# Four diagonal tiles for the first four head pairs, and two averages of v earlier in VectorE's order

## The chip, the cores and the metric

The kernel runs on one core of a Trainium2 chip. The metric is the device time of one execution in microseconds (us). TensorE (PE) multiplies matrices and loads its weights (PEld); VectorE (DVE), ScalarE (ACT) and GpSimd (POOL) do the elementwise work; SyncE (SP) issues every transfer. Each engine works through its own list of instructions in order, and the engines wait for each other by semaphores.

## The reference

Attention for 4 batches, 8 heads, 576 positions and a head size of 64, followed by two layers over the 2304 tokens:

```python
# down-sampled attention: means of 4 positions, softmax, each output repeated 4 times
q_d, k_d, v_d = (t.reshape(B, H, Sd, 4, D).mean(axis=3) for t in (q, k, v))
out_up = np.repeat(sm_attn(q_d, k_d, v_d), 4, axis=2)
# local attention: only keys with |i - j| < 4
scores = np.where(mask, scale * q @ k.T, -1e9)
out_local = softmax(scores) @ v
x = (out_up + out_local) as (2304, 512)
# first layer, 512 -> 1536 -> 512
x = (silu(x @ w_gate) * (x @ w_val)) @ w_out
# second layer, 512 -> 2048 -> 512, negative hidden values scaled by alpha
return g(x @ w_in) @ w_out2
```

## The kernel before, in words

The tokens go in 8 blocks of 288 through the attention and the first layer, then in 6 blocks of 384 through the second layer. Matrix products take each operand as a high part (rounded) and a low part (the rest), and add three products (`products`, L1005, and `outputs`, L1025). In the first layer, the attention of block j+1 is woven between the products of block j. The attention of block 0 has nothing to hide behind: it is the head of the kernel, written out by hand for each engine ("mode 0"). It takes four pairs of heads, k = 0 to 3. The change lies in this head alone.

For pair k, the head does the following:

- PE multiplies the local scores (L904) and the scores of the averaged q and k (L912, after VectorE's `average_qk`, L673).
- VectorE finds maxima and subtracts them (`local_maxima`, L697 and L701; `down_maxima`, L710 and L712). ScalarE takes the exponentials (L509, L516).
- VectorE forms the sums and their reciprocals (`reciprocals`: L718, L721, L725, the last counts `inv_ready`). GpSimd then multiplies both kinds of weights by them (`normalise`, L456 and L459; it waits for `inv_ready`).
- VectorE turns the local weights in 32 x 32 blocks into a tile `turned` that has four key groups on its diagonal and zeros elsewhere (`turn_local`, L739, four instructions). The zeros come from a memset (L659) at the start. PE transposes the averaged weights (L942), and ScalarE copies them (`copy_down_t`, L525).
- PE forms the outputs: 12 matmuls of `turned` with v's windows (L956), then 8 of the copied weights with the averaged v (L967, which counts `att_ready`). The averages of v are VectorE's for pairs 0 and 1 (`average_v`, L684) and GpSimd's for pairs 2 and 3 (L468, L470).
- VectorE adds both outputs into x (`add_up`, L748 and L750), ScalarE rounds x to its high part (L529), and the low part is GpSimd's for pairs 0 to 2 (`split_x_lo`, L474) and VectorE's for pair 3 (L755). The products of block 0 (L1005) begin when all four high and low parts are there: PE waits for GpSimd's three (`x_lo_early`, L997) and then for VectorE's (`x_lo_ready`).

Before, `turned` has two buffers for the four pairs, `turned_one` and `turned_alone`, used in turn. So VectorE's `turn_local` of pair 2 waits until PE has finished pair 0 (`att_ready` 1), and that of pair 3 until PE has finished pair 1.

What sets the order in the head is each engine's written list. VectorE's is printed in the diff below. GpSimd's is: the two weight pieces 0 and 1; `normalise(0)`; `normalise(1)`; `average_v(2)`; `normalise(2)`; `normalise(3)`; `average_v(3)`; low part of piece 2 (L437); then `split_x_lo(0)`, low part of piece 3, `split_x_lo(1)`, low part of piece 4, `split_x_lo(2)`, low part of piece 5. PE's is: scores of the four pairs; transposes 0 and 1; outputs 0; transposes 2; outputs 1; transposes 3; outputs 2; outputs 3. ScalarE's is: exponentials of the four pairs; `copy_down_t(0)`; piece 2; `copy_down_t(1)`; x high 0; `copy_down_t(2)`; piece 3; x high 1; `copy_down_t(3)`; piece 4; x high 2 and 3; piece 5.

SP issues, in this order: q and k of four pairs (`load_qk`, L293); weight pieces 0 to 2 (L304); v of four pairs, for each first the source of the averages (`load_vsrc`, L299) and then the windows (`load_vwin`, L296); pieces 3 and 4; alpha; then the refills for block 1. The source of v for block 1 goes into pair 0's buffer and waits for the first `v_averaged`; the windows wait for `att_ready`; each further weight piece j waits until piece j-3 has been split (`w_ready`).

The head's own buffers lie over the later part of the split weights `w_hi`. `EARLY_HI` pieces of `w_hi` are kept clear ahead of them; ScalarE fills the pieces behind during block 0.

Of the kernel before, what the change touches and what calls it, by code (L numbers as in the profile page):

```python
# [23 lines left out]
PAIRS = HEADS // 2  # L24
TILES = 3
TQ = TB // TILES
GROUPS = 4
GQ = TQ // GROUPS
SCORED = GQ
GK = 32  # L30
# [26 lines left out]

POOL_PIECES = 2
EARLY_PIECES = 6
EARLY_HI = 14  # L60
POOL_AVERAGES = 2
BANK = 512
STEPS1 = NB * C1
# [16 lines left out]
def build(nc, qk, vwin, vsrc, w1, w2, alpha, out, y_t):  # L80
    with ExitStack() as ctx:
        def sem(name):
            return ctx.enter_context(nc.semaphore(name))

        def sb(name, shape, dt=F32, where=ctx):
            return where.enter_context(nc.sbuf_tensor(name, shape, dt))
# [21 lines left out]
        def local_both(mode, k):  # L108
            n = scores_ps[mode][k][0]
            return ps[:, n * BANK:(n + 2) * BANK].rearrange("p (e b) -> p e b", e=2)[:, :, 0:DOWN].rearrange("p e (t c) -> p e t c", c=GK)  # L110
# [14 lines left out]
        with ExitStack() as early:  # L125
            sb("first_pieces", [128, EARLY_HI, PIECE], where=early)
            qk_early = [sb(f"qk_early{k}", [128, QK_W], where=early) for k in range(2, PAIRS)]
            vwin_early = [sb(f"vwin_early{k}", [128, TILES, 2 * HEAD], where=early) for k in range(2, PAIRS)]
            vsrc_early = [sb(f"vsrc_early{k}", [HQ, 2, 2 * HEAD, FACTOR], where=early) for k in range(1, PAIRS)]
            qk_d_early = [sb(f"qk_d_early{k}", [128, AVERAGED], where=early) for k in range(1, PAIRS)]  # L130
            v_d_early = [sb(f"v_d_early{k}", [HQ, 2, 2 * HEAD], where=early) for k in range(1, PAIRS)]
            local_early = [sb(f"local_early{k}", [128, 2 * TILES, GK], where=early) for k in range(1, PAIRS)]
            down_early = [sb(f"down_early{k}", [HQ, 2, SEQ_D], where=early) for k in range(1, PAIRS)]
            x_f32_early = [sb(f"x_f32_early{k}", [128, TB], where=early) for k in range(1, PAIRS)]
            band_tmp = sb("band_tmp", [128, GROUPS, GK], BF16, where=early)
            ident_bf = sb("ident_bf", [128, 128], BF16, where=early)
            first_max = sb("first_max", [128, PAIRS, STATS], where=early)
            first_neg = sb("first_neg", [HQ, PAIRS, 2], where=early)
            first_sum = sb("first_sum", [128, PAIRS, STATS], where=early)
            first_padded = sb("first_padded", [128, PAIRS, STATS], where=early)  # L140
            first_inv = sb("first_inv", [128, PAIRS, STATS], where=early)
# [15 lines left out]
        with ExitStack() as alone:  # L157
            turned_alone = sb("turned_alone", [128, 2 * TILES, GROUPS, GK], where=alone)
# [8 lines left out]
        with ExitStack() as att:  # L167
# [9 lines left out]
            turned_one = sb("turned_one", [128, 2 * TILES, GROUPS, GK], where=att)  # L177
# [14 lines left out]
        v_d = ([v_d_one] + v_d_early, [v_d_one] * PAIRS)  # L192
        local = ([local_one] + local_early, [local_one] * PAIRS)
        down = ([down_one] + down_early, [down_one] * PAIRS)
        turned = ([turned_one, turned_alone] * 2, [turned_one] * PAIRS)
        down_t = ([down_t_one, down_t_alone] * 2, [down_t_one] * PAIRS)
        x_f32 = ([x_f32_one] + x_f32_early, [x_f32_one] * PAIRS)

        def slot_of(k, mode):

            return k % 2 if mode else k
# [28 lines left out]
        turned_zeroed = sem("turned_zeroed")  # L230
# [16 lines left out]
        att_ready = sem("att_ready")  # L247
# [407 lines left out]

        @block.vector
        def _(dve):
            for n, buffer in enumerate((turned_one, turned_alone)):
                nc.vector.memset(buffer[:, :, :, :], 0.0).then_inc(turned_zeroed, 1)  # L659
            for mode in range(2):  # L660
                nc.vector.memset(row_sum[mode][:, :, :], 0.0).then_inc(scalars_ready, 1)
# [14 lines left out]
            def average_v(a, k):  # L676
                q = PAIRS * a + k
                mode = 0 if isinstance(a, int) and a == 0 else 1
                if mode:
                    dve.wait_ge(vsrc_in[0], 16 * (q - PAIRS) + 32)  # L680
                    dve.wait_ge(att_ready, q)
                else:
                    dve.wait_ge(vsrc_in[k], 16)
                nc.vector.tensor_reduce(v_d[mode][k][:, :, :], vsrc_sb[mode][k][:, :, :, :],  # L684
                                        AX_X, ALU.add).then_inc(v_averaged, 1)

            def local_maxima(a, k, half, mode):

                q, slot = PAIRS * a + k, slot_of(k, mode)
                dve.wait_ge(scores_ready, q + 1)  # L690
                s = local_both(mode, k)
                found = row_max[mode][:, slot, 0:2 * TILES].rearrange("p (e t) -> p e t", e=2)
                if mode:
                    b = band[:, half:half + 1, :, :].to_broadcast([128, 2, TILES, GK])
                    nc.vector.tensor_tensor(s, s, b, ALU.add).then_inc(masked, 1)
                    dve.wait_ge(masked, q - PAIRS + 1)
                nc.vector.tensor_reduce(found, s, AX_X, ALU.max).then_inc(local_max_found, 1)  # L697
                dve.wait_ge(local_max_found, q + 1)
                if mode:
                    dve.wait_ge(local_turned, GROUPS * q)  # L700
                nc.vector.tensor_tensor(local[mode][k][:, :, :].rearrange("p (e t) c -> p e t c", e=2), s,  # L701
                                        found.unsqueeze(3).to_broadcast([128, 2, TILES, GK]), ALU.subtract).then_inc(shifted, 1)

            def down_maxima(a, k, mode):

                q, slot = PAIRS * a + k, slot_of(k, mode)
                if mode:
                    dve.wait_ge(down_ready, q)
                found = row_max[mode][0:HQ, slot, 2 * TILES:STATS]
                nc.vector.tensor_reduce(found, down_both(mode, k), AX_X, ALU.max).then_inc(down_max_found, 1)  # L710
                dve.wait_ge(down_max_found, q + 1)
                nc.vector.tensor_scalar(neg_max[mode][:, slot, :], found, -SCALE / FACTOR ** 2, None, ALU.mult).then_inc(neg_max_ready, 1)  # L712

            def reciprocals(a, k, mode):

                q, slot = PAIRS * a + k, slot_of(k, mode)
                dve.wait_ge(local_ready, q + 1)
                nc.vector.tensor_reduce(row_sum[mode][:, slot, 0:2 * TILES], local[mode][k][:, :, :], AX_X, ALU.add).then_inc(summed, 1)  # L718
                dve.wait_ge(summed, q + 1)
                dve.wait_ge(down_ready, q + 1)  # L720
                nc.vector.tensor_scalar(row_padded[mode][:, slot, :], row_sum[mode][:, slot, :], 1e-9, None, ALU.add).then_inc(sum_padded, 1)  # L721
                dve.wait_ge(sum_padded, q + 1)
                if mode:
                    dve.wait_ge(down_normed, q)
                nc.vector.reciprocal(row_inv[mode][:, slot, :], row_padded[mode][:, slot, :]).then_inc(inv_ready, 1)  # L725

            def turn_local(a, k, mode):

                q = PAIRS * a + k
                dve.wait_ge(local_normed, q + 1)  # L730
                if mode:
                    dve.wait_ge(att_ready, q)
                elif k >= 2:
                    dve.wait_ge(att_ready, q - 1)
                else:
                    dve.wait_ge(turned_zeroed, 2)
                for i in range(GROUPS):
                    rows = slice(GK * i, GK * i + GK)
                    nc.vector.transpose(turned[mode][k][rows, :, i, :], local[mode][k][rows, :, :]).then_inc(local_turned, 1)  # L739
# [42 lines left out]
            down_maxima(0, 2, 0)  # L782
            reciprocals(0, 1, 0)
            turn_local(0, 0, 0)
            local_maxima(0, 3, 0, 0)
            down_maxima(0, 3, 0)
            reciprocals(0, 2, 0)
            turn_local(0, 1, 0)
            reciprocals(0, 3, 0)
            average_v(0, 0)  # L790
            turn_local(0, 2, 0)
            average_v(0, 1)
            add_up(0, 0, 0)
            turn_local(0, 3, 0)
            add_up(0, 1, 0)
# [344 lines left out]
```

## Time and profile before

| | |
|---|---|
| median of 3 runs | 978.19 us (976.51 to 978.28) |
| the profiled execution's own time | 977.23 us |
| its span in the profile | 975.2 us |
| PE busy | 948.9 us, 97% |
| PE weight loads busy | 886.3 us, 91% |
| VectorE busy | 547.8 us, 56% |
| ScalarE busy | 247.7 us, 25% |
| GpSimd busy | 138.7 us, 14% |
| largest entry in the chain of waits | PE, products at L1005, 50% |

The profile is that of one execution. Times in its rows are us from the span's start, and the second number of a timeline row is how long the row was busy. The difference of 2.0 us between its time and its span lies outside the recorded instructions.

### The profile page before, as it was taken

Reading aid. Unit: us, or ns where it says so; the run is one execution under the profiler, and the core shown is the slowest. Engines: PE = TensorE matmul, PEld = TensorE weight load, DVE = VectorE, ACT = ScalarE, POOL = GpSimd, SP = SyncE. Lnnn points to the kernel's source line nnn. Section 1 sums busy time; section 2 is a strip of 40 time slices with the busy share of each in tenths; the row PEclk is TensorE's granted clock in tenths of the full one; section 3 lists DMA queues with packets and bytes.
Section 4 is the critical chain, followed back from the end, with each engine's and each line's share of the span. In section 5 each row is a group of like instructions: output and inputs, shape, how many; then the busy total and the mean of one; then the engine's idle time right before and its main releaser. Section 6 shows DMA issues by size and latency. Waiting matters only on the chain.

```text
span 975.2 us, 20383 instructions
## 1 busy us (share of the span) xinstructions
PE 948.9 (97%) x7912; PEld 886.3 (91%) x7912; DVE 547.8 (56%) x1166; ACT 247.7 (25%) x631; POOL 138.7 (14%) x158
## 2 busy tenths in 40 slices
PE   4799999999999999999999999999999999999998
PEld 3789999899998999999999999999999999999997
DVE  7677666665765767666663544445445444444433
ACT  2455222222222222222224531111111111111111
POOL 6677010010000000010104840000000000000000
PEclk9999999999999999999999999999999999999999
DMA  8465212211211322222106530010010100100000
GB/s 257 130 193 167 85 58 60 83 53 48 94 48 41 94 66 70 59 66 72 43 10 198 163 101 1 1 66 1 0 65 0 64 1 0 65 0 0 32 0 32
DMA packets 31735, 63.06 MB, mean 65 GB/s; under 512 B 2993, under 2 KB 14257, under 8 KB 31665
## 3 DMA queue, kind: packets, MB, share of 16 engines
q1 hardware_dynamic: 31664, 62.02, 20.7%
q8 instruction: 57, 0.93, 0.4%
q14 instruction: 14, 0.11, 0.0%
HBM read 52.57 MB, written 9.44 MB: 64 GB/s over the span
## 4 chain that ended last, share of the span: by engine, by line
PE 90%; DVE 3%; POOL 2%; DMA 2%; issue 1%; ACT 1%; SPq 0%; DVEq 0%; ACTq 0%; POOLq 0%
PE ps L1005 50%; PE ps L1042 20%; PE ps L1025 14%; PE ps L956 2%; PE ps L904 1%; POOL w_lo L437 1%; DMA w_raw<-w 1%; PE ps L912 1%; PE ps L967 1%; PE ps L942 1%; DMA qk<-qk 0%; DVE x_lo L755 0%; DVE qk_d_early L673 0%; DVE turned_one L739 0%; DVE turned_alone L739 0%
## 5 line engine op out<-in xcount | busy, mean ns | idle before, releaser
L1005 PE MATMUL ps<-x_hi,w_hi 128*128 128x288 f32 x768 | 232.9, 303 | 5.8 <-issue 3.2
L1005 PE MATMUL ps<-x_lo,w_hi 128*128 128x288 f32 x768 | 227.1, 296 | 0.0
L1005 PE MATMUL ps<-x_hi,w_lo 128*128 128x288 f32 x768 | 226.4, 295 | 0.0
L579 ACT CAST h_hi<-hidden 128x288 fp32r<-128x288 f32 (+1 forms) x192 | 90.8, 473 | 404.4 <-DVE hidden L869 331.9
L832 DVE TENSOR_TENSOR h_lo<-hidden,h_hi 128x288 fp32r<-128x288 f32 (+1 forms) x192 | 112.5, 586 | 75.8 <-ACT h_hi L579 72.5
L1005 PEld LDWEIGHTS ps<-x_hi,w_hi 128*128 128x128 f32 x768 | 144.4, 188 | 10.2 <-issue 3.6
L867 DVE TENSOR_SCALAR gated<-ps,alpha_sb 128x384 f32<-128x384 f32 x96 | 59.3, 618 | 159.4 <-PE ps L1005 159.4
L1005 PEld LDWEIGHTS ps<-x_hi,w_lo 128*128 128x128 f32 x768 | 144.9, 189 | 0.0
L1005 PEld LDWEIGHTS ps<-x_lo,w_hi 128*128 128x128 f32 x768 | 144.8, 189 | 0.0
L1025 PE MATMUL ps<-h_hi,w_hi 128*128 128x288 f32 x384 | 115.5, 301 | 0.1
L1042 PE MATMUL ps<-w_lo,h_hi 128*128 128x512 f32 x288 | 113.2, 393 | 0.0
L1042 PE MATMUL ps<-w_hi,h_lo 128*128 128x512 f32 x288 | 113.2, 393 | 0.0
L1025 PE MATMUL ps<-h_hi,w_lo 128*128 128x288 f32 x384 | 112.8, 294 | 0.0
L1025 PE MATMUL ps<-h_lo,w_hi 128*128 128x288 f32 x384 | 112.7, 294 | 0.0
L1042 PE MATMUL ps<-w_hi,h_hi 128*128 128x512 f32 x288 | 112.2, 389 | 0.4 <-DVE h_lo L832 0.4
L437 POOL TENSOR_TENSOR w_lo<-w_raw,w_hi 128x512 fp32r<-128x512 f32 x68 | 90.2, 1338 | 43.7 <-ACT w_hi L574 27.4
L842 DVE SCALAR_TENSOR_TENSOR gated<-gated,ps 128x288 f32<-128x288 f32 x96 | 43.4, 452 | 90.9 <-ACT gated L604 90.9
L604 ACT ACTIVATE gated<-ps 128x288 f32<-128x288 f32 x96 | 39.4, 410 | 175.5 <-PE ps L1005 175.4
L847 DVE SCALAR_TENSOR_TENSOR hidden<-gated,ps 128x288 f32<-128x288 f32 x96 | 43.6, 454 | 52.0 <-PE ps L1005 50.7
L1025 PEld LDWEIGHTS ps<-h_hi,w_hi 128*128 128x128 f32 x384 | 72.1, 188 | 0.6 <-issue 0.6
L1025 PEld LDWEIGHTS ps<-h_lo,w_hi 128*128 128x128 f32 x384 | 72.2, 188 | 0.0
L1025 PEld LDWEIGHTS ps<-h_hi,w_lo 128*128 128x128 f32 x384 | 72.1, 188 | 0.0
(127 smaller groups left out, 1424.4 us busy)
## 6 DMA issues: line engine op xcount, KB each, us to landing
w_raw<-w SPq DMA_DIRECT2D x68, 256.0 KB, 2.7
qk<-qk SPq DMA_DIRECT2D x30, 436.0 KB, 3.4
vsrc_one<-vsrc SPq DMA_DIRECT2D x29, 288.0 KB
vwin<-vwin SPq DMA_DIRECT2D x30, 192.0 KB, 2.3
y_t<-y_sb SPq DMA_DIRECT2D x8, 576.0 KB, 3.4
x_raw<-y_t SPq DMA_DIRECT2D x6, 768.0 KB, 5.6
out<-y_sb SPq DMA_DIRECT2D x5, 768.0 KB, 4.0
qk_early<-qk SPq DMA_DIRECT2D x2, 436.0 KB, 6.4
```

Of the source, the lines that this page charges most:

```text
L437: nc.gpsimd.tensor_tensor(w_lo[:, at, :], raw, w_hi[:, at, :].bitcast(F32), ALU.subtract).then_inc(w_ready, 1)
L579: nc.scalar.copy(h_hi[r][:, 0:width], hidden[r][:, 0:width]).then_inc(h_hi_ready, 1)
L604: nc.scalar.activation(gated[:, 0:TB], gate_ps, ACT.Tanh, scale=0.5).then_inc(tanh_ready, 1)
L832: nc.vector.tensor_tensor(h_lo[r][:, 0:width], hidden[r][:, 0:width], h_hi[r][:, 0:width].bitcast(F32), ALU.subtract).then_inc(h_lo_ready, 1)
L842: nc.vector.scalar_tensor_tensor(out=gated[:, 0:TB], in0=gated[:, 0:TB], scalar=1.0, in1=gate_ps, op0=ALU.add, op1=ALU.mult).then_inc(gate ...
L847: nc.vector.scalar_tensor_tensor(out=hidden[r][:, 0:TB], in0=gated[:, 0:TB], scalar=0.5, in1=val_ps, op0=ALU.mult, op1=ALU.mult).then_inc( ...
L867: nc.vector.tensor_scalar(gated[:, :], pre_ps[r], 0.0, alpha_sb[:, c:c + 1], ALU.min, ALU.mult).then_inc(gated_ready, 1)
L904: last = nc.tensor.matmul(local_ps(mode, k, e)[GK * i:GK * i + SCORED, t * GK:(t + 1) * GK], qk_sb[mode][k][rows, first:first + SCORED], q ...
L956: nc.tensor.matmul(o[rows, t * TQ:(t + 1) * TQ].rearrange("p (i q) -> p i q", q=GQ), vwin_sb[mode][k][:, t, rows], turned[mode][k][:, e * ...
L1005: mm = nc.tensor.matmul(out_ps, w[:, piece, 128 * k:128 * k + 128], x_parts[low][:, k, :], start=(k == 0 and n == 0), stop=(k == KC - 1 an ...
L1025: mm = nc.tensor.matmul(y_ps[m], w[:, piece, 128 * m:128 * m + 128], (h_lo if low else h_hi)[c % 2][:, 0:TB], start=(c == 0 and n == 0), s ...
L1042: mm = nc.tensor.matmul(banks[m], (h_lo if low else h_hi)[c % 2][:, 128 * m:128 * m + 128], w[:, piece, :], start=(c == 0 and n == 0), sto ...
```

## The change

Pairs 2 and 3 get diagonal tiles of their own (`turned_early`), so `turn_local` no longer waits for `att_ready` in the head; VectorE zeroes four tiles instead of two. The two tiles of 128 x 768 f32 lie in the head's region, which now begins at piece 12 of `w_hi` instead of 14. VectorE's `average_v(0, 0)` moves from behind `reciprocals(0, 3, 0)` to right behind `turn_local(0, 0, 0)`, and `average_v(0, 1)` from behind `turn_local(0, 2, 0)` to right behind `turn_local(0, 1, 0)`. The lists of the other engines are as before.

```diff
-EARLY_HI = 14
+EARLY_HI = 12
...
+            turned_early = [sb(f"turned_early{k}", [128, 2 * TILES, GROUPS, GK], where=early) for k in range(2, PAIRS)]
...
-        turned = ([turned_one, turned_alone] * 2, [turned_one] * PAIRS)
+        turned = ([turned_one, turned_alone] + turned_early, [turned_one] * PAIRS)
...
-            for n, buffer in enumerate((turned_one, turned_alone)):
+            for buffer in turned[0]:
                 nc.vector.memset(buffer[:, :, :, :], 0.0).then_inc(turned_zeroed, 1)
...
                 if mode:
                     dve.wait_ge(att_ready, q)
-                elif k >= 2:
-                    dve.wait_ge(att_ready, q - 1)
                 else:
-                    dve.wait_ge(turned_zeroed, 2)
+                    dve.wait_ge(turned_zeroed, PAIRS)
...
             turn_local(0, 0, 0)
+            average_v(0, 0)
             local_maxima(0, 3, 0, 0)
             down_maxima(0, 3, 0)
             reciprocals(0, 2, 0)
             turn_local(0, 1, 0)
+            average_v(0, 1)
             reciprocals(0, 3, 0)
-            average_v(0, 0)
             turn_local(0, 2, 0)
-            average_v(0, 1)
             add_up(0, 0, 0)
             turn_local(0, 3, 0)
             add_up(0, 1, 0)
```

## Rows read from the trace of the kernel before

**Rows 1.** The page's head: span of the profiled execution.
```profile
span 975.2 us, 20383 instructions
```
**Rows 2.** Windows of PE: stretch, length, busy (instructions), clock, DMA share, GB/s.
```profile
40.00:330.00 290.00, 284.29 (x3099) 1.00 0.29 88
```
**Rows 3.** Timeline of PE, products of block 0: first, twelfth, and two later ones.
```profile
33.53 0.58 PE L1005 MATMUL ps<-x_hi,w_hi 128*128 128x288 f32 x1 [2.48 <-DVE x_lo L755]
...
36.30 0.44 PE L1005 MATMUL ps<-x_hi,w_lo 128*128 128x288 f32 x1
...
42.12 0.29 PE L1005 MATMUL ps<-x_hi,w_hi 128*128 128x288 f32 x1
42.26 0.29 PE L1005 MATMUL ps<-x_lo,w_hi 128*128 128x288 f32 x1
```
**Rows 4.** Timeline of VectorE, 0 to 6 us; in brackets idle time and its releaser.
```profile
1.79 0.70 DVE L659 MEMSET turned_alone<- 128x768 f32 x1
...
4.04 1.06 DVE L673 TENSOR_REDUCE qk_d_one<-qk 128x217 f32<-128x868 f32 x1 [1.48 <-DMA qk<-qk]
...
5.73 1.06 DVE L673 TENSOR_REDUCE qk_d_early<-qk 128x217 f32<-128x868 f32 x1 [0.63 <-DMA qk<-qk]
```
**Rows 5.** Timeline of VectorE, 16.5 to 25 us.
```profile
16.56 0.36 DVE L697 TENSOR_REDUCE first_max<-ps 128x6 f32<-128x192 f32 x1
...
17.70 0.17 DVE L712 TENSOR_SCALAR first_neg<-first_max 72x2 f32<-72x2 f32 x1
...
18.16 0.17 DVE L721 TENSOR_SCALAR first_padded<-first_sum 128x8 f32<-128x8 f32 x1
...
20.64 0.20 DVE L725 RECIPROCAL first_inv<-first_padded 128x8 f32<-128x8 f32 x1
20.76 1.16 DVE L684 TENSOR_REDUCE v_d_one<-vsrc_one 72x256 f32<-72x1024 f32 x1
22.92 1.57 DVE L739 STREAM_TRANSPOSE turned_one<-local_early 32x192 f32<-32x192 f32 x4 [1.00 <-PE ps L967]
24.52 1.22 DVE L684 TENSOR_REDUCE v_d_early<-vsrc_early 72x256 f32<-72x1024 f32 x1
```
**Rows 6.** Timeline of VectorE, 25 to 33.7 us.
```profile
27.16 1.57 DVE L739 STREAM_TRANSPOSE turned_alone<-local_early 32x192 f32<-32x192 f32 x4 [0.79 <-PE ps L967]
...
32.32 0.85 DVE L755 TENSOR_TENSOR x_lo<-x_f_early,x_hi 128x288 fp32r<-128x288 f32 x1 [0.50 <-ACT x_hi L529]
```
**Rows 7.** Timeline of GpSimd, 18 to 34 us.
```profile
18.76 1.04 POOL L468 TENSOR_TENSOR vsrc_early<-vsrc_early 72x512 f32<-72x512 f32 x1 [2.47 <-DMA vsrc_early<-vsrc]
19.88 0.63 POOL L470 TENSOR_TENSOR v_d_early<-vsrc_early 72x256 f32<-72x256 f32 x1
...
21.56 0.51 POOL L456 TENSOR_TENSOR local_early<-local_early,first_inv 128x192 f32<-128x192 f32 x1
...
26.91 0.79 POOL L474 TENSOR_TENSOR x_lo<-x_f,x_hi 128x288 fp32r<-128x288 f32 x1 [1.27 <-ACT x_hi L529]
...
30.04 0.80 POOL L474 TENSOR_TENSOR x_lo<-x_f_early,x_hi 128x288 fp32r<-128x288 f32 x1 [1.04 <-ACT x_hi L529]
...
32.07 0.79 POOL L474 TENSOR_TENSOR x_lo<-x_f_early,x_hi 128x288 fp32r<-128x288 f32 x1
32.89 1.42 POOL L437 TENSOR_TENSOR w_lo<-w_raw,w_hi 128x512 fp32r<-128x512 f32 x1
```
**Rows 8.** Timeline of all engines at 10.5 us: GpSimd and VectorE side by side.
```profile
10.53 1.26 POOL L437 TENSOR_TENSOR w_lo<-w_raw,w_hi 128x512 fp32r<-128x512 f32 x1
10.75 1.07 DVE L721 TENSOR_SCALAR first_padded<-first_sum 128x8 f32<-128x8 f32 x1
```
**Rows 9.** Transfers issued in 5.8 to 6.3 and 6.8 to 7.2 us: KB, us to landing.
```profile
vwin<-vwin SPq DMA_DIRECT2D x1, 192.0 KB, 9.0
...
vwin<-vwin SPq DMA_DIRECT2D x1, 192.0 KB, 10.2
```
**Rows 10.** Timeline of all engines: the weight pieces 5 and 6 being issued.
```profile
25.67 3.68 SPq L304 DMA_DIRECT2D w_raw<-w x2
```

## The prediction, made before the changed kernel ran

> **What bounds the kernel now.** I read the page first. The span is 975.2 us [rows 1]. The windows of PE come next: between 40 and 330 us PE is busy for 284.29 of 290 us [rows 2], so behind the head PE sets the time, and a head that ends earlier or later moves all that follows. What the change can be worth is therefore when the products of block 0 start. That is the first row of PE's timeline: 33.53 us, after 2.48 us idle, released by VectorE's low part of pair 3 [rows 3]. That part ended at 32.32 + 0.85 = 33.17 [rows 6], 0.36 us ahead of the matmul. GpSimd's third low part ended at 32.07 + 0.79 = 32.86 [rows 7]. So two engines end the head, and the second is only 0.31 us ahead of the first. That margin matters more here than VectorE's idle time.
>
> VectorE's timeline shows what the change aims at: 1.00 us idle before the turn of pair 2 and 0.79 us before that of pair 3, both released by PE's outputs [rows 5, 6]. From the turn of pair 3 on the head is one chain: the turn ends at 28.73 (27.16 + 1.57) and, with the 0.03 us that separate 22.92 + 1.57 from 24.52 [rows 5], at 28.76 VectorE adds up pair 1, ScalarE rounds it and then copies the weights of pair 3, PE forms the outputs of pair 3, VectorE adds them up, and the low part follows. From 28.76 to 33.17 that is 4.41 us, which moves as a whole.
>
> **The change, part by part.**
>
> Two more memsets: 2 x 0.70 = 1.40 us and two short gaps on VectorE [rows 4]. What hides them is the wait of 1.48 us for q and k at 4.04. At most some 0.15 us sticks out, and the next wait of 0.63 us for a transfer swallows that [rows 4]. Cost: nothing. Moving the region by two pieces costs nothing either: those pieces are written by ScalarE inside block 0, well behind 33.53.
>
> The two waits for a free tile go: up to 1.00 + 0.79 = 1.79 us of VectorE's time. The averages are only moved, so VectorE's work until pair 1 is added up is the same. Without other waits that step would begin at 28.76 - 1.79 = 26.97, and VectorE's last low part would end at 33.17 - 1.79 = 31.4.
>
> The first moved average starts at 16.56, where pair 3's maxima began [rows 5]. Its data are there: the windows of pair 0, issued behind its source on the same queue, landed 9.0 us after an issue before 6.3, so by 15.3; those of pair 1 by 7.2 + 10.2 = 17.4, ahead of the second average [rows 9]. It takes 1.16 us, and everything behind it on VectorE is that much later: pair 3's maxima, the exponentials that ScalarE does before any copy, and the reciprocals of pair 2. The second average (1.16 to 1.22 us [rows 5]) delays the reciprocals of pair 3 further. These were ready at 20.64 + 0.20 = 20.84; now 20.84 + 1.16 + 1.22 = 23.22 at the earliest.
>
> **Who waits for that** is GpSimd's normalise of pair 3, which began at 21.56 [rows 7]. With less than 0.1 us for the signal (an estimate, from the gaps of that size between instructions) it can begin at 23.3, 1.74 us later. Behind it in GpSimd's list stand the average of pair 3, piece 2 and the three low parts that PE needs. On the way GpSimd has two idle stretches, 1.27 and 1.04 us, both for ScalarE's rounding [rows 7], which itself comes earlier or no later. They absorb 2.31 us. So GpSimd's third low part would end at 32.86 + 1.74 - 2.31 = 32.29, and it, not VectorE, would be last.
>
> **The port between VectorE and GpSimd** decides the rest. VectorE's scalar step L721, 0.17 us elsewhere [rows 5], took 1.07 us at 10.75 and ended at 11.82, just behind GpSimd's subtraction that ran from 10.53 to 11.79 [rows 8]. After the move, the same kind of step for pair 3 (L712) comes at 17.70 + 1.16 = 18.86 [rows 5]. GpSimd's first step of the average of pair 2 starts at 18.76, released by a transfer, and runs until 19.80 [rows 7]. The transfer does not move, so L712 runs into it and ends at about 19.82 instead of 19.03: 0.80 us. L721 then comes at about 20.1, beside GpSimd's second step, which ends at 19.88 + 0.63 = 20.51 [rows 7]: another 0 to 0.35, I take 0.3. That is the likeliest course: VectorE's chain moves by 1.79 - 1.1 = 0.7 us to the front, the last low part of VectorE ends near 32.5, and the reciprocals of pair 3 come at 23.22 + 1.1 = 24.3. Normalise starts at 24.4, 2.8 us late, 0.5 more than the 2.31 us absorb. GpSimd's third low part then ends at 32.86 + 0.5 = 33.4. VectorE's low part (two SBUF inputs) falls beside these steps; where they met before, GpSimd's next subtraction took 1.42 us against 1.26 [rows 7, 8], so 0 to 0.2 more. With 0.36 us until the matmul the products start at 33.7 to 33.9, 0.2 to 0.4 us later than before; with the lower bound of every term (0.6 of port waits) they start at 33.2. I take +0.3 us.
>
> The Trainium skill (SBUF — State Buffer, Who interferes with whom) says that issue order, not the op's shape, decides who blocks. L712 is only 0.10 us behind GpSimd's step by the sum above. If the transfer lands 0.1 us later, L712 goes first, and by that rule GpSimd loses only the short step; that is rival B.
>
> **Transfers.** The source of v for block 1 waits for the first average to read its buffer, and is now issued about 4.2 us earlier (20.76 to 16.56 [rows 5]). It lies behind the early transfers on one queue, so it delays no load of the head. Piece 5 was issued at 25.67 [rows 10], when piece 2 had been split; GpSimd splits that up to 2.8 us later, so it is issued at 28.5. It still lands ahead of its use, which is ScalarE's last copy of the head, behind the high part of pair 3 (before 32.32). With the 3.68 us of that row for both pieces, 32.2 for the second is the worst. Cost: nothing, and up to 0.3 if the cover fails.
>
> **The clock at the start.** The first products are slow: 33.53 to 36.30 for eleven steps is 0.25 us each, the lower level (1.2 GHz), against 0.14 at 42.12, the upper (2.4 GHz) [rows 3]; PE had mostly idled before. If the rise comes at the same moment, whatever the start, a shift of the start counts only 0.14 / 0.25 = 0.56.
>
> **The sum.** 977.23 for the profiled execution + 0.3 = 977.5. The median of the runs is 0.96 above that execution, the lowest run 0.72 below it; I put the forecast at 977.8, between the sum and the same sum made on the median. A measurement of this kernel can tell some 0.2%, 1.96 us, from no change; nothing above comes near it.
>
> **The rivals.**
> A, the forecast (0.52): GpSimd ends the head, start between 33.2 and 33.9, no change that can be told; 977.8.
> B (0.25): L712 gets the port first. GpSimd loses 0.17 us, and only L721 stands, for about 0.4. Normalise of pair 3 starts at 23.7, 2.1 us late, inside the 2.31 that are absorbed; GpSimd ends at 32.7 to 32.9, VectorE at 31.8, products at 33.05 to 33.3. That is 0.2 to 0.5 us gained against before, 0.65 less than A: 977.15. For it speaks the margin of 0.10 us, against it that L712 is behind in the sum.
> C (0.12): the idle time of VectorE is all gained, because GpSimd takes its waits elsewhere or meets no port wait. Bounds: 31.4 + 0.36 gives 31.76, a gain of 1.77 us; with GpSimd last at 32.29 it is 0.9 us. Against the 977.5 that stands for no change in the forecast that is 975.7 to 976.6, and with a low run under it faster by more than 1.96 us. Against it speaks GpSimd's order, where `normalise(3)` stands ahead of all three low parts.
> D, slower (0.11): the late normalise costs nearly its full amount and the clock rises late. Place: GpSimd's row at 21.56 [rows 7]. If only its idle 1.27 absorbs and not the 1.04, its third low part ends at 32.86 + 2.8 - 1.27 = 34.4, and the products start at 34.8, 1.2 us slower; with 1 us more at the lower level of the clock, which costs 1 - 0.56 = 0.44, that is 1.7 us: 979.2. It decides from the point where ScalarE's rounding of pair 1 moves back together with GpSimd. To pass 1.96 the clock would have to stay low for 1.8 us more. Against it: VectorE adds up pair 1 earlier, not later.
>
> **How the numbers follow.** The range holds A and B with the spread of the runs (976.51 to 978.28, so 0.9 to either side of their middle), the nearer part of C, and D to its price: 976.0 to 979.3. Faster by over 0.2% takes C and a low run, or part of B with one: 0.08. Slower by over 0.2% takes D and more: 0.05. Within: 0.87.
>
> **What would show it.** Right: no idle before the turns of pairs 2 and 3; L712 of pair 3 at 18.8 to 18.9 with about 0.9 us; reciprocals of pair 3 at about 24; GpSimd idle before `normalise(3)` and next to none before its low parts; PE's first product released by GpSimd's L474, at 33.2 to 33.9; from there on the trace as before. Wrong: the first product still released by VectorE, or before 32.8; L712 at 0.17 us (then B or C); an idle stretch of PE behind 40 us that was not there.

## The result, and the profile after

The changed kernel takes 980.08 us (median of 13 runs, 979.24 to 982.92), the kernel before 978.33 us (median of 13, 976.51 to 979.97). The ratio is 1.0019, with a 95% interval of 1.0011 to 1.0028: it is slower, by some 1.9 us (by the ratio; the medians differ by 1.75). The forecast was no change, with a range that ended at 979.3.

The page's head and parts of its costliest groups; [rows 1] answers to the first line.

```profile
span 979.6 us, 20385 instructions
PE 951.7 (97%) x7912; PEld 888.0 (91%) x7912; DVE 552.9 (56%) x1168; ACT 247.9 (25%) x631; POOL 138.7 (14%) x158
...
L1004 PE MATMUL ps<-x_hi,w_hi 128*128 128x288 f32 x768 | 233.7, 304 | 10.2 <-DVE x_lo L754 6.0
```

The last line shows where to look: PE's products waited 6.0 us for VectorE's low part of x, where before that wait was 2.48 us [rows 3]. The lines of the changed kernel are numbered otherwise: L754 is before's L755, L1004 is L1005, L738 is L739, and on GpSimd L469, L475 and L438 are L468, L474 and L437.

VectorE's timeline in the head, to be set beside [rows 5, 6]:

```profile
15.14 1.53 DVE L738 STREAM_TRANSPOSE turned_one<-local_one 32x192 f32<-32x192 f32 x4
16.70 1.22 DVE L685 TENSOR_REDUCE v_d_one<-vsrc_one 72x256 f32<-72x1024 f32 x1
...
18.97 0.21 DVE L713 TENSOR_SCALAR first_neg<-first_max 72x2 f32<-72x2 f32 x1
...
19.47 0.43 DVE L722 TENSOR_SCALAR first_padded<-first_sum 128x8 f32<-128x8 f32 x1
...
23.33 0.20 DVE L726 RECIPROCAL first_inv<-first_padded 128x8 f32<-128x8 f32 x1
23.45 1.53 DVE L738 STREAM_TRANSPOSE turned_early<-local_early 32x192 f32<-32x192 f32 x4
25.01 0.23 DVE L747 TENSOR_SCALAR up<-ps 128x72 f32<-128x72 f32 x1
25.28 0.46 DVE L749 TENSOR_TENSOR x_f<-ps,up 128x288 f32<-128x288 f32 x1
25.66 1.56 DVE L738 STREAM_TRANSPOSE turned_early<-local_early 32x192 f32<-32x192 f32 x4
27.25 0.23 DVE L747 TENSOR_SCALAR up<-ps 128x72 f32<-128x72 f32 x1
...
29.85 0.46 DVE L749 TENSOR_TENSOR x_f_early<-ps,up 128x288 f32<-128x288 f32 x1
30.81 4.36 DVE L754 TENSOR_TENSOR x_lo<-x_f_early,x_hi 128x288 fp32r<-128x288 f32 x1 [0.50 <-ACT x_hi L530]
```

Both idle stretches ahead of the turns are gone. Pair 1 is added up at 27.25 instead of 28.77, and the low part of pair 3 is ready to go at 30.81 instead of 32.32. So far the change does what it says: it brings the last step 1.5 us forward. That step then takes 4.36 us instead of 0.85. The instruction ahead of it (29.85), of the same size but with only one of its two inputs in SBUF, took its usual 0.46 us beside GpSimd's work.

GpSimd's timeline, to be set beside [rows 7], shows what stood beside it:

```profile
18.12 1.03 POOL L469 TENSOR_TENSOR vsrc_early<-vsrc_early 72x512 f32<-72x512 f32 x1 [1.69 <-DMA vsrc_early<-vsrc]
...
23.61 0.51 POOL L457 TENSOR_TENSOR local_early<-local_early,first_inv 128x192 f32<-128x192 f32 x1 [2.27 <-DVE first_inv L726]
...
29.64 0.79 POOL L475 TENSOR_TENSOR x_lo<-x_f_early,x_hi 128x288 fp32r<-128x288 f32 x1
30.39 1.27 POOL L438 TENSOR_TENSOR w_lo<-w_raw,w_hi 128x512 fp32r<-128x512 f32 x1
31.62 0.79 POOL L475 TENSOR_TENSOR x_lo<-x_f_early,x_hi 128x288 fp32r<-128x288 f32 x1
32.37 2.48 POOL L438 TENSOR_TENSOR w_lo<-w_raw,w_hi 128x512 fp32r<-128x512 f32 x2
```

The normalise of pair 3 starts at 23.61, 2.05 us later than before, and after it GpSimd has no idle stretch left until 32.37 + 2.48 = 34.85. VectorE's low part ends at 30.81 + 4.36 = 35.17, 0.32 us behind that. Before, GpSimd's third low part ended at 32.86, and VectorE's ended at 33.17, 0.31 us behind it [rows 6, 7].

PE's timeline, to be set beside [rows 3]:

```profile
35.52 0.58 PE L1004 MATMUL ps<-x_hi,w_hi 128*128 128x288 f32 x1 [5.98 <-DVE x_lo L754]
...
40.66 0.34 PE L1004 MATMUL ps<-x_hi,w_lo 128*128 128x288 f32 x1
40.84 0.29 PE L1004 MATMUL ps<-x_hi,w_hi 128*128 128x288 f32 x1
```

The first product comes 1.99 us later, which is about the measured difference. This one profiled execution took longer than the median (981.4 us), its span is 4.4 us over that of before, and the clock explains part of the rest. The products of 0.44 us, the lower level, went on until 40.8, 5.3 us from the first one, against less than 4.4 us before (they took 0.29 us, the upper level, from 37.87). At the start of a later block the changed kernel was 3.1 us behind (313.62 against 310.51), after PE had idled there for 2.23 us against 1.43. Then this execution had one more stretch at the lower level, here beside the same stretch of before:

```profile
313.70:317.00 3.30, 3.30 (x16) 0.52 0.02 5
```
```profile
313.70:317.00 3.30, 3.30 (x27) 1.00 0.03 5
```

These are windows of PE (length, busy time, instructions, granted clock, DMA share, GB/s). At 0.52 of full speed PE did 16 products in 3.3 us where it did 27 before, so the stretch costs some 1.3 us (an estimate from these two rows), which completes the 4.4. Nothing makes it a cost of the change: 5 of the 13 runs of the changed kernel report a mean clock below 1, and so do 24 of the 74 runs of the kernel before that were taken beside the experiments (an outlier of 2055.99 us left out).

### The profile page after: what moved, and what is told of

The parts are those of the page before. It is cut to its first block, busy times and chain, and to the rows that moved or that the text cites. A ratio compares the mean times of both kernels' runs of the same rounds, so it can differ in the third digit from the quotient of the medians.

```text
span 979.6 us, 20385 instructions
## 1 busy us (share of the span) xinstructions
PE 951.7 (97%) x7912; PEld 888.0 (91%) x7912; DVE 552.9 (56%) x1168; ACT 247.9 (25%) x631; POOL 138.7 (14%) x158
## 4 chain that ended last, share of the span: by engine, by line
PE 89%; DVE 4%; POOL 2%; DMA 2%; issue 2%; ACT 1%; SPq 0%; DVEq 0%; ACTq 0%; POOLq 0%
PE ps L1004 50%; PE ps L1041 20%; PE ps L1024 14%; PE ps L955 2%; POOL w_lo L438 1%; PE ps L903 1%; DMA w_raw<-w 1%; PE ps L911 1%; DVE x_lo L754 1%; PE ps L966 1%; PE ps L941 1%; DMA qk<-qk 0%; DVE h_lo L831 0%; DVE qk_d_early L674 0%; DVE turned_early L738 0%
## 5 line engine op out<-in xcount | busy, mean ns | idle before, releaser
L1004 PE MATMUL ps<-x_hi,w_hi 128*128 128x288 f32 x768 | 233.7, 304 | 10.2 <-DVE x_lo L754 6.0
L1004 PE MATMUL ps<-x_lo,w_hi 128*128 128x288 f32 x768 | 227.9, 297 | 0.0
L1004 PE MATMUL ps<-x_hi,w_lo 128*128 128x288 f32 x768 | 227.0, 296 | 0.0
L1004 PEld LDWEIGHTS ps<-x_hi,w_hi 128*128 128x128 f32 x768 | 145.0, 189 | 14.8 <-issue 10.5
L1004 PEld LDWEIGHTS ps<-x_hi,w_lo 128*128 128x128 f32 x768 | 145.6, 190 | 0.0
L1004 PEld LDWEIGHTS ps<-x_lo,w_hi 128*128 128x128 f32 x768 | 145.4, 189 | 0.0
L438 POOL TENSOR_TENSOR w_lo<-w_raw,w_hi 128x512 fp32r<-128x512 f32 x68 | 90.3, 1341 | 46.2 <-ACT w_hi L575 27.4
```

Of the source, the lines that this page charges most:

```text
L438: nc.gpsimd.tensor_tensor(w_lo[:, at, :], raw, w_hi[:, at, :].bitcast(F32), ALU.subtract).then_inc(w_ready, 1)
L1004: mm = nc.tensor.matmul(out_ps, w[:, piece, 128 * k:128 * k + 128], x_parts[low][:, k, :], start=(k == 0 and n == 0), stop=(k == KC - 1 an ...
```

## The experiments

The stated theory P was this. A VectorE instruction with two SBUF inputs (the low part) needs a port that GpSimd holds, and while GpSimd works on without a gap it does not get it. The moved averages delay GpSimd's normalise of pair 3 by 2 us and so close GpSimd's gaps. All ratios below are against the kernel before, run on the same chip. They need not equal the ratio of the two medians.

The head's own time differs between executions before it comes to anything that was edited, so a second measure is used for it: the time from the first turn (pair 0's, the STREAM_TRANSPOSE of `turned_one`) to the first product. It is 33.53 - 14.99 = 18.54 us in the kernel before and 35.52 - 15.14 = 20.38 us in the changed one, 1.84 more. The row of before:

```profile
14.99 1.53 DVE L739 STREAM_TRANSPOSE turned_one<-local_one 32x192 f32<-32x192 f32 x4
```

**Each part alone.** First the tiles without the moves (the edit is to the changed kernel):

```diff
             turn_local(0, 0, 0)
-            average_v(0, 0)
             local_maxima(0, 3, 0, 0)
...
             turn_local(0, 1, 0)
-            average_v(0, 1)
             reciprocals(0, 3, 0)
+            average_v(0, 0)
             turn_local(0, 2, 0)
+            average_v(0, 1)
             add_up(0, 0, 0)
```

> Only the four tiles; the averages of v stay where they were. Theory P (the port): the changed kernel is slower because VectorE's low part of pair 3 falls where GpSimd works through piece 4, the low part of pair 2 and piece 5 without a gap, and gets no turn at the port they share until GpSimd runs dry. That pile-up comes from GpSimd's normalise of pair 3 being 2 us late, which comes from the moved averages. Here normalise of pair 3 starts near 21.6 us as before, VectorE adds up pair 1 near 27.1, and its low part of pair 3 takes under 1.4 us; the first product is at 31.8 to 32.5, and the time is 1 to 2 us under the kernel before. Rival Q (the tiles): the tiles themselves (more zeroing, or their place in memory) bring the stretch of 4.4 us; then it shows here too, and the time is 1.5 to 2 us over before.

Measured: 977.08 us, ratio 0.9966 (0.9954 to 0.9978), so faster than before by some 3.3 us by the ratio, and by 2.0 us by the medians (979.09 for before, with six runs of this kernel). The timeline of all engines in this kernel:

```profile
14.35 1.53 DVE L738 STREAM_TRANSPOSE turned_one<-local_one 32x192 f32<-32x192 f32 x4
...
20.57 1.16 DVE L685 TENSOR_REDUCE v_d_one<-vsrc_one 72x256 f32<-72x1024 f32 x1
20.73 0.51 POOL L457 TENSOR_TENSOR local_early<-local_early,first_inv 128x192 f32<-128x192 f32 x1 [0.34 <-DVE first_inv L726]
...
29.90 0.80 POOL L475 TENSOR_TENSOR x_lo<-x_f_early,x_hi 128x288 fp32r<-128x288 f32 x1
30.33 0.68 DVE L754 TENSOR_TENSOR x_lo<-x_f_early,x_hi 128x288 fp32r<-128x288 f32 x1 [0.50 <-ACT x_hi L530]
30.89 2.51 POOL L438 TENSOR_TENSOR w_lo<-w_raw,w_hi 128x512 fp32r<-128x512 f32 x2 [0.20 <-ACT w_hi L537]
...
31.36 0.58 PE L1004 MATMUL ps<-x_hi,w_hi 128*128 128x288 f32 x1 [2.30 <-DVE x_lo L754]
```

GpSimd normalises pair 3 at 20.73, comes to its third low part at 29.90, and has a gap of 0.20 us ahead of piece 5. VectorE's low part takes 0.68 us, and the first product is at 31.36. The tiles are not what costs. The start is 2.17 us ahead of before, but 0.64 us of that was there at the first turn (14.35 against 14.99). From there on the tiles are worth 1.53 us (17.01 us to the first product against 18.54). Part of the lead is given back in block 0, where PE waits for x_f three times (0.58, 0.38, 0.58 us at 50.6, 68.0 and 85.8 us) against once for 0.30 before; behind it the lead is 95.44 against 96.73, 1.3 us. The chain of waits leads from these stops over ScalarE's piece copies to the transfers of the weight pieces. The timed gain is more than this pair of profiles shows, and where the rest is stays open; the profile of before was of a short execution (977.23 us, against that median of 979.09).

ScalarE's copy of piece 5 shows where the gap of 0.20 us comes from, here in the kernel before, the changed kernel and this one:

```profile
32.20 1.13 ACT L536 CAST w_hi<-w_raw 128x512 fp32r<-128x512 f32 x2
```
```profile
30.68 0.61 ACT L537 CAST w_hi<-w_raw 128x512 fp32r<-128x512 f32 x1
```
```profile
30.20 1.13 ACT L537 CAST w_hi<-w_raw 128x512 fp32r<-128x512 f32 x2
```

GpSimd's part of piece 5 needs this copy. Before and with the tiles alone it started 0.69 us after the copy's start (32.89 and 30.89), when its third low part had ended 0.03 and 0.20 us earlier (32.86 and 30.70): GpSimd was ahead of ScalarE and had to stop. In the changed kernel the copy comes 1.5 us earlier than before and the third low part only 0.45 us (32.41), so GpSimd finds piece 5 ready and does not stop.

Then the moves without the tiles, which is the new order of VectorE's list in the kernel before:

> Only the two averages moved; two tiles as before. Theory P: PE has finished pairs 0 and 1 before VectorE comes to turn pairs 2 and 3, so the tiles are not waited for; the head runs as in the changed kernel, VectorE's low part of pair 3 takes 3 to 4.5 us, the first product is at 35.0 to 35.6, and the time is 1.3 to 2.3 us over before. Rival Q: without the tiles the low part of pair 3 takes under 1.4 us and the time is within 0.7 us of before.

Measured: 980.84 us, ratio 1.0015 (1.0005 to 1.0026). The same stretch of VectorE and PE:

```profile
30.18 4.19 DVE L755 TENSOR_TENSOR x_lo<-x_f_early,x_hi 128x288 fp32r<-128x288 f32 x1 [0.50 <-ACT x_hi L529]
...
34.72 0.58 PE L1005 MATMUL ps<-x_hi,w_hi 128*128 128x288 f32 x1 [5.82 <-DVE x_lo L755]
```

The loss is there with only two tiles. The first product (34.72) is 0.3 us ahead of the band that was expected, because the first turn came early (14.65); from the turn on it is 20.07 us, 1.53 more than before. So the moved averages cost what the change costs, and with them in place the tiles bring nothing: PE is done with pairs 0 and 1 before VectorE wants their tiles. The times of the two kernels cannot be told apart (1.0015 and 1.0019).

**A gap for VectorE.** Three kernels leave the changed kernel as it is and make GpSimd wait for VectorE's low part of pair 3, by a semaphore of its own (`x_lo_last`, which PE waits for too). The first puts that wait ahead of piece 5, the second one instruction earlier:

```diff
             for k in range(PAIRS - 1):
                 split_x_lo(k)
+                if k == PAIRS - 2:
+                    pool.wait_ge(x_lo_last, 1)
                 split_rest(3 + k)
```

> The changed kernel, but GpSimd starts the split of piece 5 only when VectorE's low part of pair 3 is done (a semaphore of its own); all else as changed. Theory P: the low part starts at 30.8, is let in when GpSimd ends its low part of pair 2 at 32.4, and ends at 32.9 (some 2.0 us long instead of 4.4); the first product is at 33.2, and the time falls by 2.2 to 3 us against the changed kernel, to 0 to 1 us under before. Rival R (the stretch has another cause, such as the transfers or ScalarE beside it): it stays over 3.5 us long and the first product stays at 35.5 or later.

```diff
             for k in range(PAIRS - 1):
+                if k == PAIRS - 2:
+                    pool.wait_ge(x_lo_last, 1)
                 split_x_lo(k)
                 split_rest(3 + k)
```

> The changed kernel, but GpSimd waits one instruction earlier than in the run where piece 5 waited: its low part of pair 2 starts when VectorE's low part of pair 3 is done. Theory P: VectorE's is let in at the first gap of GpSimd, so it is as long as the distance to that gap. It starts at 30.2 to 30.8 while GpSimd splits piece 4, and that ends at 31.1 to 31.7: it takes 1.3 to 1.4 us, against 1.9 with the gap one instruction later and 4.4 without. GpSimd's low part of pair 2 follows, and the first product is at 32.7 to 33.3. Rival R' (VectorE is let in by chance, or by the age of its request): its length does not follow the gap.

Measured: 978.17 us, ratio 0.9993 (0.9984 to 1.0003), and 979.5 us, ratio 0.9995 (0.9984 to 1.0006). The timeline of the first:

```profile
29.79 1.30 POOL L439 TENSOR_TENSOR w_lo<-w_raw,w_hi 128x512 fp32r<-128x512 f32 x1
30.22 1.93 DVE L757 TENSOR_TENSOR x_lo<-x_f_early,x_hi 128x288 fp32r<-128x288 f32 x1 [0.50 <-ACT x_hi L533]
31.01 0.82 POOL L476 TENSOR_TENSOR x_lo<-x_f_early,x_hi 128x288 fp32r<-128x288 f32 x1
...
32.23 2.51 POOL L439 TENSOR_TENSOR w_lo<-w_raw,w_hi 128x512 fp32r<-128x512 f32 x2 [0.40 <-DVE x_lo L757]
32.85 0.58 PE L1008 MATMUL ps<-x_hi,w_hi 128*128 128x288 f32 x1 [3.90 <-DVE x_lo L757]
```

and of the second:

```profile
29.67 1.26 POOL L439 TENSOR_TENSOR w_lo<-w_raw,w_hi 128x512 fp32r<-128x512 f32 x1
30.08 1.17 DVE L757 TENSOR_TENSOR x_lo<-x_f_early,x_hi 128x288 fp32r<-128x288 f32 x1 [0.50 <-ACT x_hi L533]
31.33 0.79 POOL L476 TENSOR_TENSOR x_lo<-x_f_early,x_hi 128x288 fp32r<-128x288 f32 x1 [0.40 <-DVE x_lo L757]
...
32.71 0.58 PE L1008 MATMUL ps<-x_hi,w_hi 128*128 128x288 f32 x1 [3.90 <-POOL x_lo L476]
```

The low part's length follows the gap. It ends 0.32 us behind GpSimd's last instruction each time: 32.15 against 31.83, 31.25 against 30.93, 35.17 against 34.85 in the changed kernel. This shows that GpSimd's unbroken work is what holds it; that it does so by the shared port is theory P's reading, which the undisturbed instruction at 29.85 with one SBUF input bears out. And it takes the loss away: the first product comes at 32.85 and 32.71, and both intervals of the ratio include 1. The second kernel also shows GpSimd as the last to end the head: its low part ends at 32.12, and PE starts 0.59 us later, not the 0.36 that it takes behind VectorE's low part.

The third kernel gives GpSimd a better order as well:

```diff
-            for k in range(PAIRS - 1):
-                split_x_lo(k)
-                split_rest(3 + k)
+            split_x_lo(0)
+            split_rest(3)
+            split_x_lo(1)
+            split_x_lo(2)
+            pool.wait_ge(x_lo_last, 1)
+            split_rest(4)
+            split_rest(5)
```

> The changed kernel with GpSimd's order low part 0, piece 3, low part 1, low part 2, then (when VectorE's low part of pair 3 is done) pieces 4 and 5. Theory P: GpSimd's third low part ends at 31.2 instead of 32.4, VectorE's starts at 30.8 and ends at 31.7, the first product is at 32.0, 1.5 us ahead of before; the time is 1 to 2.5 us under before. Rival R: the low part of pair 3 is still over 3.5 us long, no gain on the changed kernel.

Measured: 977.86 us, ratio 0.9982 (0.9971 to 0.9993). VectorE's low part takes 0.71 us and the first product is at 31.56. At 88.28 PE then stops for 2.31 us, and the chain leads to a weight piece whose transfer took 5.49 us.

**How much of the averages is too much.** Four tiles, and only the first average moved:

> Four tiles and only the first average of v moved up, behind the first turn; the second stays. Theory P: the reciprocals of pair 3 and GpSimd's normalise of pair 3 come 1.1 to 1.5 us later than with the tiles alone, of which GpSimd's idle time before its low parts (0.84 and some 0.4 us) takes most. It ends close to gapless: VectorE's low part of pair 3 takes either under 1.4 us (a gap is left before piece 5) and the first product is at 31.4 to 32.3, or over 3 us and it is at 34 or later. In both cases no faster than the tiles alone. Rival S (the averages are worth moving, only both are too much): 0.3 us or more under the tiles alone.

Measured: 977.15 us, ratio 0.9972 (0.9961 to 0.9984). The low part takes 0.68 us (31.00), the first product is at 32.04, inside the first of the two expected courses. One moved average is still absorbed, and it gains nothing: from the first turn (14.83) to the first product it is 17.21 us, against 17.01 for the tiles alone. That speaks against rival S; the intervals of the two ratios overlap, so the times alone would not decide it.

**Better than both?** The tiles alone with the wait of piece 5, and the tiles alone with GpSimd's better order:

> Four tiles, averages where they were, and GpSimd's piece 5 waiting for VectorE's low part of pair 3. Theory P: with the tiles alone GpSimd already had a gap ahead of piece 5 (0.20 us), so nothing is left to gain in the head: low part of pair 3 at 0.5 to 0.8 us, first product at 31.2 to 31.5, time within 0.7 us of the tiles alone. Rival T (GpSimd's piece 5 still costs there): 0.5 us or more earlier than 31.36.

> Four tiles, averages where they were, GpSimd's low part of pair 2 ahead of piece 4, pieces 4 and 5 behind VectorE's low part of pair 3. Theory P: VectorE's low part is alone at the port (0.45 us from 30.33), the first product is at 31.1, 0.2 us ahead of the tiles alone. Behind the head the weight pieces come 1 to 2 us later than with the tiles alone, and PE waits for them in block 0, as it did with a single idle of 2.3 us at 88 us in the changed kernel with this order: the time is 0 to 1.5 us over that of the tiles alone. Rival V (weights are no limit behind the head): 0.2 us or more under it.

Measured: 976.87 us, ratio 0.9975 (0.9966 to 0.9985), and 976.09 us, ratio 0.9965 (0.9951 to 0.9979). In the second the low part takes 0.46 us from 30.37 and the first product is at 31.53, so the reorder does not bring it ahead of the 31.36 of the tiles alone (a step of VectorE at 16.65 lost 0.64 us to GpSimd there, so this one profile is no clean comparison), and the times of the two cannot be told apart (0.9965 and 0.9966), which decides neither for P nor for V. All three versions with the tiles and the averages in their old place beat both kernels, and their intervals overlap; the simplest, the tiles alone, is the one to keep. In the first of these two the first product came at 33.00, 1.64 us behind the tiles alone and well outside what was expected, for reasons ahead of the edit. At the first turn 0.62 us of it was there (14.97 against 14.35). Another 0.85 us came in these rows of VectorE and of GpSimd:

```profile
17.68 1.02 DVE L716 TENSOR_SCALAR first_neg<-first_max 72x2 f32<-72x2 f32 x1
```
```profile
17.64 1.04 POOL L470 TENSOR_TENSOR vsrc_early<-vsrc_early 72x512 f32<-72x512 f32 x1 [1.38 <-DMA vsrc_early<-vsrc]
```

GpSimd's average of pair 2, released by its transfer, went first by 0.04 us, and VectorE's step of 0.17 us took 1.02. This is the collision that the prediction put on L712, in another kernel. It depends on when a transfer lands (17.64 here, 18.12 in the changed kernel, 18.76 before), so such a step can move the head by 0.85 us from one execution to the next.

**What lets VectorE in.** In the blocks behind the head, the changed kernel's VectorE does get the port between two GpSimd instructions that follow each other without a gap:

```profile
55.23 2.76 POOL L438 TENSOR_TENSOR w_lo<-w_raw,w_hi 128x512 fp32r<-128x512 f32 x2 [1.94 <-ACT w_hi L537]
55.52 1.31 DVE L754 TENSOR_TENSOR x_lo<-x_f,x_hi 128x288 fp32r<-128x288 f32 x1 [1.90 <-ACT x_hi L530]
```

The same instruction takes 1.31 us there, and GpSimd's two take 2.76 us instead of the 2.48 of the head. Three kernels asked what differs. One put a tiny memset between piece 4 and the low part of pair 2:

```diff
+                if k == PAIRS - 2:
+                    nc.gpsimd.memset(band_tmp[:, 0:1, 0:1], 0.0)
                 split_x_lo(k)
```

> The changed kernel with one tiny GpSimd memset (128 x 1, it only writes) between piece 4 and its low part of pair 2. Open: why VectorE is let in at some changes from one GpSimd instruction to the next and not at others; in the head it lost five of five without a gap, in the later blocks it got the next one each time. Theory G (a gap, or an instruction that reads nothing, is enough): VectorE's low part gets its turn at the memset and takes 1.1 to 1.4 us; GpSimd's low part of pair 2 follows, first product at 32.5 to 33.3. Theory H (in the head it gets in only when GpSimd really stops): 4.1 to 4.5 us as in the changed kernel, first product at 34.7 to 35.7.

Measured: 980.37 us, ratio 1.0017 (1.0008 to 1.0027).

```profile
30.26 1.26 POOL L438 TENSOR_TENSOR w_lo<-w_raw,w_hi 128x512 fp32r<-128x512 f32 x1
30.67 4.40 DVE L756 TENSOR_TENSOR x_lo<-x_f_early,x_hi 128x288 fp32r<-128x288 f32 x1 [0.50 <-ACT x_hi L532]
31.47 0.10 POOL L486 MEMSET band_tmp<- 128x1 bf16 x1
```

The memset passed and VectorE was not let in. The second gave pair 3 the x tile of the later blocks, the third put another VectorE instruction ahead of the low part:

```diff
-        x_f32 = ([x_f32_one] + x_f32_early, [x_f32_one] * PAIRS)
+        x_f32 = (x_f32_early + [x_f32_one], [x_f32_one] * PAIRS)
```

> The changed kernel with pair 3's x in the tile that the later blocks use, and pair 0's in one of the head's. Theory J (it is the place of VectorE's operand that makes the head different from the later blocks): its low part is let in at the next change of instruction, 0.8 to 1.4 us. Theory H: no difference, 4.1 to 4.5 us.

```diff
-            split_x_lo(3, 0, 3, 0)
             average_qk(1, 0)
+            split_x_lo(3, 0, 3, 0)
```

> The changed kernel with VectorE's average of q and k for block 1 ahead of its low part of pair 3, where VectorE was idle for 0.5 us. Theory P: the request comes some 0.5 us later, while GpSimd is at piece 4 or its low part of pair 2, and still waits for GpSimd to run dry at 34.0 to 34.9: low part 2.7 to 3.9 us, first product within 0.4 us of the changed kernel's. Rival K (what stands behind the low part in VectorE's list holds it up): under 1.4 us.

Measured: 980.54 us, ratio 1.0023 (1.001 to 1.0036), low part 4.37 us; and 983.13 us, ratio 1.004 (1.0021 to 1.0058), low part 3.98 us. Both of these last kernels show the long wait, so neither the tile's place nor what follows the low part on VectorE is the reason. With the tile swapped the first product came at 34.31, but its first turn had come at 14.16; from there it is 20.15 us, about as in the changed kernel (20.38). The length of the third is just over the band of theory P, and it ended 0.31 us behind GpSimd again (34.87 against 34.56). By the ratios it cost 2.1 us more than the changed kernel, though its first product (35.23) is no later. It had three runs, and the intervals overlap. Its profile shows where time went in that execution: in block 0 PE waited 3.3 us for x_f (1.04, 0.42 and 1.84 us), where the changed kernel's waited for none, and a stretch at half the clock followed the last of these waits:

```profile
91.40 0.47 PE L911 MATMUL ps<-qk_d_one 64*72 64x144 f32 x4 [1.84 <-DVE x_f L749]
```
```profile
93.00:96.30 3.30, 3.30 (x16) 0.50 0.74 234
```

All three runs report a mean clock below 1. Whether the edit brings these waits on or the executions happened to have them was not tested. What makes VectorE lose each change of instruction in the head and win it in the later blocks stays open.

## Why the prediction was wrong

**The forecast's sum.** It was 977.5 from the profile, put at 977.8; measured 980.08. The sum had the products start 0.3 us later, so its direction was right; they started 1.99 us later and the time rose by 1.9 us, six times the sum's term.

**What held.** The memsets cost next to nothing (the first average of q and k at 4.20 instead of 4.04, the first turn at 15.14 instead of 14.99). The data of both averages were there. Both idle stretches went. GpSimd's normalise of pair 3 was named as the step that waits: 23.61, against 24.4 in case A and 23.7 in case B, and its idle stretches were eaten as forecast. The port waits of L712 and L721 (now L713 and L722) were 0.04 and 0.26 us, together 0.30 and not 1.1, because the transfer landed 0.64 us earlier; that is near case B. GpSimd's third low part ended at 31.62 + 0.79 = 32.41, between its lower bound of 32.29 and B's 32.7. VectorE was ready for its low part at 30.81. By the forecast's own count the products would have started at 32.8 to 33.0, some 0.6 us ahead of before.

**The step that failed** is the sentence on the port at the end of the head: "VectorE's low part (two SBUF inputs) falls beside these steps; where they met before, GpSimd's next subtraction took 1.42 us against 1.26 [rows 7, 8], so 0 to 0.2 more." It priced the meeting for GpSimd alone, and let VectorE's low part move along at the 0.85 us that it had before, inside the 4.41 us "which moves as a whole". It took 4.36 us, 3.51 more than counted, and 3.9 more than the 0.46 it takes with GpSimd idle (in the tiles-only kernel with the better order). The row to read it from was there: VectorE's low part took 0.85 us at 32.32 [rows 6], nearly twice its free length, and ended 0.31 us behind GpSimd's instruction. The prediction went on to say that GpSimd would be last, and it did not ask what GpSimd had queued behind its third low part: pieces 5 and 6, two more readers of SBUF for 2.48 us, which it now reached when ScalarE's copies were done. The experiments with the gap show this as the cause; with a gap put back, the start falls by 2.7 us (35.52 to 32.85). One of the prediction's own signs of being wrong is what the trace shows: the first product was still released by VectorE.

The Trainium skill (SBUF — State Buffer, Who interferes with whom) says that a VectorE instruction with two SBUF inputs contends with a GpSimd instruction that reads SBUF, and that the loser fully blocks. The trace of before agrees (0.85 us instead of 0.46, until GpSimd's instruction ended). In the changed kernel VectorE's instruction was held not by one GpSimd instruction but until four had run (30.39 to 34.85); here the measurement decides.

**The rivals.** B was right for the middle of the head (pair 3's normalise at 23.61 against its 23.7), though the collision was missed because the transfer came earlier, not later. C did not come true for the changed kernel, but it is about what the tiles give without the moves: from the first turn on 1.53 us less than before, between its two gains of 0.9 and 1.77 us. D had the right sign for another reason: neither GpSimd's lost 1.04 nor a late clock was the cause, though the clock did stay low longer in the profiled execution.

**The transfers.** Piece 5 was issued at 27.72 instead of 25.67, and nothing of the head waited for it, as forecast.

## What to carry to other kernels

When an engine ends a stage with an instruction that another engine's work can hold up, cost it with everything that the other engine has queued and ready, not with one instruction: in this head it was all of it, in the later blocks one. Work put ahead of the step that feeds GpSimd can close the gaps in GpSimd's list, and in this head those gaps were what let VectorE in. When a change has two parts, run each alone: here one part gained 3.3 us by the ratios and the other turned it into a loss of 1.9. And before a head's start is compared between two single profiles, look whether they already differed ahead of the edit.

## What was not expected of the hardware

VectorE's subtraction with two SBUF inputs waited until four GpSimd instructions in a row had ended, and took 4.36, 4.19, 4.40, 4.37 and 3.98 us in five kernels, where it takes 0.46 us alone and 1.3 us behind one GpSimd instruction in the later blocks. A GpSimd memset of 0.10 us between did not let it in; a real stop of GpSimd did, each time, and in the kernel before one of 0.03 us (32.86 to 32.89) seems to have been enough. The products' first stretch at the lower clock differs from profile to profile, and not by how late the products start: the thirteenth product followed the first after 4.11 us before (start at 33.53), after 4.50 in the changed kernel (35.52), and after 4.17 in the one with the memset (35.42).
